# Group sums as one product a tile, turn and slots of kv as one product, and both halves of y for two experts as one

## What is computed

```python
kv = np.einsum('bhsd,bhse->bhde', k, v)
out = np.einsum('bhsd,bhde->bhse', q, kv)
rms = np.sqrt(np.mean(out * out, axis=-1, keepdims=True) + 1e-06)
x = out / rms * g_norm                    # then laid out as 4608 x 512
logits = x @ phi                          # 32 slots
d = np.exp(logits - logits.max(0));  d /= d.sum(0) + 1e-09
slot_input = d.T @ x                      # 32 x 512, 4 slots per expert
for e in range(E):
    slot_out[e] = np.maximum(slot_input[e] @ w1[e], 0.0) @ w2[e]
c = np.exp(logits - logits.max(1));  c /= c.sum(1) + 1e-09
return c @ slot_out
```

## Time and profile before

| | us |
|---|---|
| median of 3 runs (171.91 to 172.02) | 171.94 |
| the profiled execution | 172.04 |
| its span, from the first to the last instruction | 170.7 |
| PE busy | 151.3 |
| VectorE busy | 86.6 |
| ScalarE busy | 89.0 |
| GpSimd busy | 59.6 |
| bytes moved by DMA | 71.65 MB, 420 GB/s over the span |

### The profile page before, as it was taken

One profiled execution on the slowest core, in us unless ns is written; L12 is line 12 of the kernel. 1 busy time (PEld: TensorE's weight loads), 2 busy tenths in 40 slices (PEclk: granted clock), 3 DMA queues, 4 the chain that ended last, 5 costly groups with the idle time before them and its releaser, 6 DMA issues.

```text
span 170.7 us, 4234 instructions
## 1 busy us (share of the span) xinstructions
PE 151.3 (89%) x1832; PEld 105.5 (62%) x1832; DVE 86.6 (51%) x185; ACT 89.0 (52%) x230; POOL 59.6 (35%) x73
## 2 busy tenths in 40 slices
PE   7989697989999899999899998989999989998700
PEld 3469576979778878897697674346665543345300
DVE  1122156284677266762946698823888137205700
ACT  3036576796975886859759864202223045205700
POOL 7000707638357745377382679500000004000000
PEclk9999999999999999999999999999999999699965
DMA  5999999999999999999999999999999999999988
GB/s 190 414 429 423 443 418 440 465 422 454 449 418 434 431 428 430 418 409 449 422 434 422 434 407 426 443 428 420 430 426 438 451 418 407 420 432 410 405 380 369
DMA packets 4365, 71.65 MB, mean 420 GB/s; under 512 B 790, under 2 KB 790, under 8 KB 922
## 3 DMA queue, kind: packets, MB, share of 16 engines
q1 hardware_dynamic: 3994, 71.18, 97.8%
q0 software_dynamic: 352, 0.20, 0.4%
HBM read 61.94 MB, written 9.44 MB: 418 GB/s over the span
## 4 chain that ended last, share of the span: by engine, by line
PE 59%; DMA 13%; ACT 12%; DVE 7%; SPq 2%; issue 1%
PE psum L214 59%; DMA arena<-in_kv_dram 13%; ACT bd L214 3%; ACT sq L214 3%; ACT xall L214 2%; SPq L214 2%; DVE arena L214 1%; DVE logits L214 1%; ACT arena L214 1%; DVE ms L214 1%; ACT part L214 1%; ACT d L214 1%; DVE part L214 1%; ACT r L214 1%; DVE acc L214 1%
## 5 line engine op out<-in xcount | busy, mean ns | idle before, releaser
L214 PE MATMUL psum<-bd,arena 128*128 128x192 f32 (+1 forms) x320 | 56.1, 335 | 1.9 <-ACT bd L214 1.5
L214 PEld LDWEIGHTS psum<-bd,arena 128*128 128x128 f32 (+1 forms) x320 | 45.4, 179 | 8.6 <-ACT bd L214 2.8
L214 DVE TENSOR_REDUCE ms<-sq 128x16 f32<-128x1024 f32 (+1 forms) x19 | 22.1, 1163 | 32.5 <-ACT sq L214 32.3
L214 POOL TENSOR_TENSOR part<-part,r 128x512 f32<-128x512 f32 x17 | 17.8, 1048 | 49.7 <-DVE r L214 49.7
L214 POOL TENSOR_TENSOR xall<-xall,r 128x512 f32<-128x512 f32 x34 | 34.7, 1042 | 0.0
L214 ACT ACTIVATE sq<-psum 128x512 f32<-128x512 f32 x36 | 21.5, 598 | 11.6 <-PE psum L214 11.3
L214 PEld LDWEIGHTS psum<-arena 128*64 128x64 f32 (+1 forms) x640 | 19.0, 137 | 8.3 <-DMA arena<-in_kv_dram 3.2
L214 PE MATMUL psum<-arena 128*64 128x64 f32 (+1 forms) x640 | 21.7, 226 | 2.2 <-DMA arena<-in_kv_dram 2.2
L214 ACT COPY xall<-psum 128x512 f32<-128x512 f32 x34 | 20.6, 606 | 0.0
L214 ACT COPY part<-psum 128x256 f32<-128x256 f32 (+1 forms) x38 | 13.6, 359 | 12.9 <-DVE part L214 11.7
L214 DVE TENSOR_REDUCE logits<-part 128x64 f32<-128x512 f32 (+1 forms) x18 | 17.8, 990 | 0.0
(11 more groups left out here) (80 smaller groups left out, 124.8 us busy)
## 6 DMA issues: line engine op xcount, KB each, us to landing
arena<-in_w_dram SPq DMA_DIRECT2D x4, 4096.0 KB, 23.5
arena<-in_w_dram SPq DMA_DIRECT2D x4, 2048.0 KB, 20.0
arena<-in_t_dram SPq DMA_DIRECT2D x1, 6912.0 KB, 36.0
arena<-in_w_dram SPq DMA_DIRECT2D x2, 3072.0 KB, 22.7
arena<-in_kv_dram SPq DMA_DIRECT2D x2, 2304.0 KB, 23.5
arena<-in_kv_dram SPq DMA_DIRECT2D x1, 4608.0 KB, 42.6
arena<-in_kv_dram SPq DMA_DIRECT2D x1, 3584.0 KB, 32.1
arena<-in_kv_dram SPq DMA_DIRECT2D x3, 1152.0 KB, 12.0
```

Source lines behind the costliest of these rows:

```text
L214: inst = getattr(engine, method)(*args, **kwargs)
```

## The change

- `group_sum` now takes four tiles a call (and then two), with one product of 512 columns a tile, on 32 columns of the array. The columns of ones are gone. In their place, in the first call of a group, VectorE sums d over the six tiles (`total`, in the buffer of `diag`), TensorE multiplies that by a column of ones (32x1) into the PSUM bank of tag "m", and VectorE adds the result to a column of `small`. The rest of the call, the products with x, stands behind this on TensorE.
- `slots` of kv multiplies once by `turns`, which holds `ident` and gphi side by side (256 columns), where it turned and multiplied apart. The output lies in two banks, one for each pair.
- `acc` has 512 columns on 128 partitions; folding it takes four products with `sel` instead of two with `fold`.
- experts 0 and 1 make both halves of y in one product of 512 columns, right behind their h; ScalarE copies the sum of the two (`gather_whole`), and each `mix` adds two more products for it.
- in the tail the first call of group 4's sum stands behind `products(Z)`, and `fill_wide` writes into another tile.

```diff
     def slots(self, gs):
             kvT = [self.kvT[:, k].rearrange("p w d -> p (w d)") for k in range(len(gs))]
             for t, g in zip(kvT, gs):
-                nc.tensor.transpose(self.pT[:, g], t, ident)
-            for t, g in zip(kvT, gs):
-                nc.tensor.matmul(self.pM[:, g], lhsT=t, rhs=gphi[:, g], start=True, stop=True)
+                nc.tensor.matmul(self.turned[:, g], lhsT=t, rhs=turns[:, : g + 2 : g + 1], start=True, stop=True)
...
+    def add_up(G, part, new):
+        if G == 0:
+            nc.vector.tensor_copy(out=part, in_=new)
+        else:
+            nc.vector.scalar_tensor_tensor(
+                out=part, in0=part, scalar=alphas[G][: part.shape[0]], in1=new, op0=ALU.mult, op1=ALU.add
+            )
+
     def group_sum(G, i):
 
+        n = GROUPS[G]
         if i == 0:
-            sums[G] = ps.tile([P, 258], F32, tag="s", name=f"pS{G}")
+            total = wk.tile([P, NS], F32, tag="diag", name=f"total{G}")
+            nc.vector.tensor_reduce(out=total, in_=ds[G].rearrange("p t n -> p n t"), axis=AX.X, op=ALU.add)
+            p1 = ps.tile([P, P], F32, tag="m", name=f"p1{G}")[:NS, 64:65]
+            nc.tensor.matmul(p1, lhsT=total, rhs=ones[:, :1], start=True, stop=True)
+            add_up(G, small[:NS, 4:], p1)
+            sums[G] = ps.tile([P, 512], F32, tag="s", name=f"pS{G}")
         pS = sums[G]
-        for a in range(2):
-            x = xts[(g0[G] + i + a) % NX]
-            for j in range(2):
-                at = 64 * a + 32 * j
-                nc.tensor.matmul(
-                    pS[at : at + 32].rearrange("p (j n) -> p j n", n=129),
-                    lhsT=ds[G][:, i + a],
-                    rhs=x[:, j::2],
-                    start=i == 0,
-                    stop=i == GROUPS[G] - 2,
-                )
...
+        for t in range(i, min(i + 4, n)):
+            at = 32 * (t % 4)
+            nc.tensor.matmul(
+                pS[at : at + 32],
+                lhsT=ds[G][:, t],
+                rhs=xts[(g0[G] + t) % NX].rearrange("p j n -> p (j n)"),
+                start=i == 0,
+                stop=t + 4 >= n,
+            )
+        if i + 4 >= n:
+            add_up(G, acc, pS)
...
     oZ = products(Z)
+    group_sum(*todo_sums.pop(0))
     root(s - 1, tail_ps[:, 0, 256 : 256 + H])
...
-    for j in range(2):
+    for j in range(4):
         nc.tensor.matmul(
-            psT[:, 64 * j : 64 * j + 64], lhsT=acc[:, 129 * j : 129 * j + 128], rhs=fold[:, 0], start=True, stop=True
+            psT[:, 32 * j : 32 * j + 32], lhsT=acc[:, P * j : P * j + P], rhs=sel[:, 0], start=True, stop=True
         )
...
-    def expert_y(e, hf, cs=range(8)):
+    def expert_y(e, hf=None):
...
+            if hf is None:
+                rhs = homes("w2", e)[0].rearrange("p (f n) -> p f n", f=2)[:, :, c * 256 : c * 256 + 256]
+                out = pY[32 * j : 32 * j + 32, 0].rearrange("p (f n) -> p f n", f=2)
...
+        for ready in (True, False):
+            for f in range(2):
+                y = y_whole[:, (2 * hf + f) * P : (2 * hf + f + 1) * P] if ready else ys[hf][f]
+                nc.tensor.matmul(pz[f], lhsT=sel.rearrange("p a n -> p (a n)"), rhs=y, start=ready, stop=not ready)
...
-    expert_y(0, 0)
+    expert_y(0)
...
-    expert_y(1, 0)
+    expert_y(1)
+    gather_whole()
...
-    expert_y(0, 1)
-    expert_y(1, 1)
```

More of the change, by code:

```diff
@@ L296, in soft_moe_linear_attention @@
     g2 = arena[:, 128:129]
-    xall = const.tile([P, NX, 4, 129], F32, name="xall")
+    xall = const.tile([P, NX, 4, P], F32, name="xall")
     xflat = xall.rearrange("p i j n -> p (i j n)")
@@ L362, in soft_moe_linear_attention @@
     nc.scalar.preload_act_table_set("natural_log_exp_and_others")
-    ident = const.tile([P, P], F32, name="ident")
+    turns = const.tile([P, 3, P], F32, name="turns")
+    ident = turns[:, 0]
     make_identity(nc, ident)
@@ L367, in soft_moe_linear_attention @@
     nc.gpsimd.memset(ones, 1.0)
-    zeros = const.tile([P, 256], BF16, name="zeros")
+    zeros = const.tile([P, P], BF16, name="zeros")
     nc.vector.memset(zeros, 0.0)
     stepped = const.tile([P, 16], F32, name="stepped")
-    small = const.tile([P, 4], F32, name="small")
+    small = const.tile([P, 5], F32, name="small")
     eps = small[:, :1]
     nc.gpsimd.memset(eps, EPS_RMS)
-    fold = const.tile([P, 2, 64], F32, name="fold")
-    nc.vector.tensor_reduce(out=fold[:, 0], in_=ident.rearrange("p (g n) -> p n g", g=2), axis=AX.X, op=ALU.add)
     sel = const.tile([P, 4, NS], F32, name="sel")
@@ L378, in soft_moe_linear_attention @@
     nc.gpsimd.tensor_copy(out=sel[:, 1:], in_=sel[:, :1].to_broadcast([P, 3, NS]))
-    gphi = const.tile([P, 2, 2, 2, NS], F32, name="gphi")
+    gphi = turns[:, 1:].rearrange("p g (h i n) -> p g h i n", h=2, i=2)
     nc.gpsimd.memset(gphi, 0.0)
@@ L387, in soft_moe_linear_attention @@
         nc.gpsimd.memset(bds[i], 0.0)
-    nc.gpsimd.memset(xall[:, :, :, 128:129], 1.0)
-    nc.gpsimd.tensor_copy(out=fold[:, 1], in_=fold[:, 0])
     xts = [xall[:, (i + 6) % NX] for i in range(NX)]
@@ L397, in soft_moe_linear_attention @@
     run_max = [small[:, 1 + i : 2 + i] for i in range(2)]
-    acc = const.tile([P, 258], F32, name="acc")
+    acc = const.tile([P, 512], F32, name="acc")
     def pool(**tags):
@@ L413, in __init__ @@
             self.pkv = t[:, :, :128].rearrange("p w (g d) -> p w g d", g=2)
-            self.pT = t[:, 0, 128:384].rearrange("p (g n) -> p g n", g=2)
-            self.pM = t[:, 1, 128:384].rearrange("p (g h w n) -> p g h w n", g=2, h=2, w=2)
+            self.turned = t[:, :, 128:384].rearrange("p g (a n) -> p g a n", a=2)
+            self.pT = t[:, :, 128:256]
+            self.pM = t[:, :, 256:384].rearrange("p g (h w n) -> p g h w n", h=2, w=2)
         def products(self, r):
@@ L760, in soft_moe_linear_attention @@
         if T in sums_at:
-            todo_sums += [(sums_at[T], i) for i in range(0, GROUPS[sums_at[T]], 2)]
+            todo_sums += [(sums_at[T], i) for i in range(0, GROUPS[sums_at[T]], 4)]
         if todo_sums:
@@ L779, in soft_moe_linear_attention @@
     group_exp(G - 1)
-    todo_sums += [(G - 1, i) for i in range(0, GROUPS[G - 1], 2)]
+    todo_sums += [(G - 1, i) for i in range(0, GROUPS[G - 1], 4)]
     mean_square(s - 1)
     oZ = products(Z)
+    group_sum(*todo_sums.pop(0))
     root(s - 1, tail_ps[:, 0, 256 : 256 + H])
@@ L797, in soft_moe_linear_attention @@
     load_w("w1", 7)
-    fill_wide(ps.tile([P, 512], F32, tag="m", name="fill"), LATE_FILL[0])
+    fill_wide(tail_ps[:, 1], LATE_FILL[0])
     group_max_T(G)
@@ L807, in soft_moe_linear_attention @@
     fill(LATE_FILL[2], home=tail_ps[:, 1], cols=512)
-    for i in range(0, GROUPS[G], 2):
+    for i in range(0, GROUPS[G], 4):
         group_sum(G, i)
@@ L815, in soft_moe_linear_attention @@
     psT = ps.tile([P, P + 1], F32, tag="m", name="psT")
-    for j in range(2):
+    for j in range(4):
         nc.tensor.matmul(
-            psT[:, 64 * j : 64 * j + 64], lhsT=acc[:, 129 * j : 129 * j + 128], rhs=fold[:, 0], start=True, stop=True
+            psT[:, 32 * j : 32 * j + 32], lhsT=acc[:, P * j : P * j + P], rhs=sel[:, 0], start=True, stop=True
         )
     nc.tensor.matmul(
-        psT[:, 128:129], lhsT=fold.rearrange("p a n -> p (a n)"), rhs=acc[:, 128:129], start=True, stop=True
+        psT[:, 128:129], lhsT=sel[:NS].rearrange("p a n -> p (a n)"), rhs=small[:NS, 4:], start=True, stop=True
     )
@@ L864, in soft_moe_linear_attention @@
     hTs = {}
+    whole = NE - LATE
+    y_whole = xall[:, 8].rearrange("p j n -> p (j n)")
     pY = ps.tile([P, 2, 512], F32, tag="y", name="pY", bufs=1)
     def w2_unit(e, hf):
[L868 to L871, removed]
+        return whole + hf * LATE // 2 + (e - whole) // 2, 8 * (e % 2)
     def expert_h(e):
@@ L889, in expert_h @@
         nc.vector.transpose(out=hTs[e].rearrange("p c n -> p (c n)"), in_=h)
-    def expert_y(e, hf, cs=range(8)):
-        u, at = w2_unit(e, hf)
-        for c in cs:
+    def expert_y(e, hf=None):
+        for c in range(8):
             j = c % 4
[L895 to L901, removed]
+            if hf is None:
+                rhs = homes("w2", e)[0].rearrange("p (f n) -> p f n", f=2)[:, :, c * 256 : c * 256 + 256]
+                out = pY[32 * j : 32 * j + 32, 0].rearrange("p (f n) -> p f n", f=2)
+            else:
+                u, at = w2_unit(e, hf)
+                rhs = w_block("w2", u, at + c)
+                out = pY[32 * j : 32 * j + 32, 1 - hf, :256]
+            first, last = (0, whole - 1) if hf is None else (whole, NE - 1)
+            nc.tensor.matmul(out, lhsT=hTs[e][:, c], rhs=rhs, start=e == first and c < 4, stop=e == last and c >= 4)
     zs = {}
@@ L913, in halves, with gather_whole @@
         return t
+    def gather_whole():
+        nc.scalar.copy(y_whole, pY[:, 0])
     def gather(hf):
-        ys[hf] = halves(f"y{hf}", [pY[:, hf, f * P : f * P + P] for f in range(2)])
```

(7 more changed lines are left out.)

17 lines of the change are left out of this document (5 added, 12 removed).

## The result

The changed kernel takes 200.62 us (median of 4 runs, 200.37 to 200.99) against 171.93 us: a ratio of 1.167, 95% interval 1.166 to 1.168. The forecast was 200.7. The profiled execution took 200.99 us, with a span of 199.7. The total was met to 0.1 us, and that is in part luck: the clock's term was 4 us too small, and what made up for it were waits and sums that were priced 1 us too dear each and a half clock of before (1.7 us) that is missing after.

What follows compares the result with a forecast made beforehand. TensorE, busy without a gap, was taken to bound the kernel from 27 us on. 19.5 - 1.2 + 2.3 + 0.7 + 3.1 + 0.1 + 4.3 = 28.8 us gave 200.7 us beside the median; range 192.5 to 206.5.

Steps and rivals of the forecast that it cites:

- the clock's term: Behind the four new waits the granted clock falls to half, 1.1 us lost each: +4.3 us (0 to 6.8).
- waits: TensorE stands ahead of the 32x1 product of groups 0 to 3 until VectorE has summed d: +19.5 us.
- small waits that fall away: Earlier TensorE waits at T = 13, 27 and 31 vanish as other engines catch up in the meantime: -1.2 us.
- sums and turn, in TensorE's work: Wider rounds and 32x1 product, 0.57 a group, +2.3 us; turn and slots of kv in one product, +0.7 us.
- tail: Groups 4 and 5, their sums, wider rounds and acc's folding delay VectorE's write of the experts' inputs: +3.1 us (2 to 4).
- experts: One 512-column product for y costs as much as two of 256; two more products in each mix: +0.1 us.
- last store: At the end, the last store is issued behind the last copies as before, so nothing of it is hidden.
- A microsecond of TensorE standing still is a microsecond of the span: From 27 us on, TensorE is busy without a gap and waits for no loads, so its idling lengthens the span.
- transfers set the end: Rival: transfers take the whole span and cover TensorE's delay, so the time stays at 172 us; chance 0.03.
- instructions, not columns: Rival: a TensorE round costs 0.53 whatever its width, so the sums and slots gain: 169.3 us; chance 0.02.
- The work alone: Rival: VectorE's sum is not on TensorE's way and only the added work counts: 177 us; chance 0.02.

Runs made afterwards that it cites:

- no wait: Changed kernel with groups 0 to 3's sum over d a turn earlier on VectorE and the 32x1 product behind the group's last products: 173.53 us.
- waits filled: Changed kernel with 18 filler products on TensorE ahead of each 32x1 product of groups 0 to 3: 193.39 us.
- the wait alone: Kernel before, its sums kept, with only the sum over d and the 32x1 product added ahead of the products of groups 0 to 3: 195.36 us.
- The turn alone: Kernel before with the turn and the slots of kv in one product, nothing else: 171.94 us.
- one filler less: Changed kernel without its waits, with three instead of four float32 fillers ahead of the turned maximum in the tail: 173.80 us.
- the late output: Kernel before with ten filler products ahead of the second mix: 172.12 us, eight runs from 171.85 to 172.16, four from 173.49 to 173.62.
- half-wait run: Changed kernel with the sum over d and 32x1 product of groups 0 to 3 moved behind the group's last products, a turn later: 179.38 us.

## Why the prediction was right, and where it was not

| step | predicted, us | measured, us | from |
|---|---|---|---|
| waits | 19.5 | 18.4 | changed kernel |
| small waits that fall away | -1.2 | -1.2 | no wait, changed kernel |
| sums and turn, in TensorE's work | 3.0 | 1.8 | no wait |
| tail | 3.1 | 2.9 | no wait |
| experts | 0.1 | -0.2 | changed kernel |
| half clock behind the waits | 4.3 | 8.3 | changed kernel, waits filled |
| half clock in the first output half, gone | not in the sum | -1.7 | changed kernel |
| last store | 0 | 0.9 | changed kernel |

The measured column adds up to 29.2 us; the two spans differ by 29.0. The forecast's 28.8 is near because terms that were too large and one that was far too small happened to cancel.

**The wait** is right in mechanism, place and size. It came out of comparing two engines' lists at one turn: where TensorE stands when VectorE gets to the new instruction. The runs with the whole wait, a third of it and none gave 200.6, 179.4 and 173.5 us, and the wait alone on the kernel before 195.4.

**The sums and the turn** were too dear. The step that failed is the price of an old round in the loop: 0.53 was read from three rounds in a row in the tail, while in the loop each stands between products of another form; there the round at 62.48 was followed at

```profile
63.06 1.54 PE L214 MATMUL psum<-arena 128*64 128x64 f32 x48
```

so 0.58, and three are 1.74. The new two rounds and the small product are 0.99 + 0.89 + 0.12 = 2.00. That is 0.26 more for a group, not 0.57. And the chain is not TensorE alone: its small waits shrink by 1.2 of the 1.8 us by which its work grows. The 1.2 was right in size, but the reason given, that the others catch up during the four waits, was not: without these they fall away as well. Without the wait the tail's filler began 1.5 us later than before, of which 1.1 is the tail's own step for group 4; for four groups and six batches 0.4 remain. The turn alone takes TensorE from 55.34 to 56.20, 0.86 for a batch where the earlier trace rows show 0.67 and 0.90 was forecast, and costs the time nothing.
The Trainium skill gives 4x for the transpose mode with float32 (TensorE: Matmul & The Clock Gate, Terms); the rows of before show a factor of 2 between a transpose and a product of its width. Its advice to use transposes for turning (Perfetto Trace Analysis, Optimizing Tensor Performance) made no difference here: 171.94 us without them, 171.93 with them.

**The tail** was right in its sum: 3.4 us without the waits, less the 0.4 for the loop, against 3.1. The trace without the waits bears out the parts too: group 4's step 1.1 us (a wait of 1.30 for its sum over d where 0.66 stood before, and 0.45 more of products; 1.07 forecast), group 5's later start 0.6 (0.7), its products 0.4 (0.6), the addition to acc 0.3 (0.3), the turning 0.6 (0.5). The filler as the carrier of the delay is borne out by the trace with one filler less (0.7 us), not by its times.

**The clock** is the term that was mis-sized most. The step that failed is the range "between 0.5 and 1.7 us a wait": it took the one dip's 3.4 us for the length of every dip. (Four of its 1.1 are 4.4, not 4.3, which changes nothing.) That part of the dip lies in the wait was true three times in four, but two of the four lasted 6.8 us, and behind each wait TensorE worked at half clock for 2.9 to 6.3 us; that is 1.4 to 3.2 us a wait at most, 2.1 on average by the 8.3. The fillers showed it on the chip: the tail 8.3 us earlier with the waits left in place, and 7.2 us less in the time.

**What bounds the kernel** was half right. "A microsecond of TensorE standing still is a microsecond of the span" holds for the delays: in the changed kernel the last copy of the result comes 28.0 us later, and the end 29.0. It doesn't hold for gains: with results 1.8 us earlier the time stays 171.9. The rival "transfers set the end" is thus true of the kernel before, for up to 1.8 us, and was put too low as a statement about it; for a delay of 28 us it decides nothing. No kernel tried here beats the one before.

**The dip gone and the last store** were not in the sum. The half clock at 146.7 to 150.1 of before is missing in the changed kernel's profile; it is absent with the turn alone too, whose output is that of before, and the late output's two clusters fit a dip that comes and goes between runs. So it is likely no effect of the edit that could have been forecast; no two traces of one kernel show it. The last store took 9.6 us instead of 8.7, with nothing loading beside it; in the other kernels it took from 8.7 to 10.5. Why in this one stays open.

Of the rivals, "instructions, not columns" is refuted for these shapes: half as many products with x, and a group's sum costs 0.26 us more, 0.12 of it for the 32x1 product. The Trainium skill's rule that larger matmuls are more efficient than smaller ones (Perfetto Trace Analysis, Optimizing Tensor Performance) did not show in this case, by the same 0.26. "The work alone" would have been 173.5, not 177.

## What to carry to other kernels

A product that reads what another engine makes is placed by that engine's list, not by its own size: before moving work to a second engine, find what stands ahead of the new instruction there in the same turn, and put the product that needs it behind all work that doesn't. Price a round of small products from rows in the place where it will stand, not from a run of them. When a kernel sits where transfers and computing end together, lateness shows and earliness, up to a point, doesn't; ask which side of that point an edit moves it to.

## What was not expected of the hardware

A TensorE wait of 1.6 to 1.9 us left the granted clock at full (the half-wait run), and waits of 4.2 to 4.9 us brought it to half four times in four, for 3.4 or 6.8 us, once only after TensorE had begun to work again. Filler products of zeros held it at full through the same waits (waits of 0.3 to 1.0 us remained).
